# Rest tokens of v ahead of the fourth row tile, and a ring of four PSUM bank pairs for the u and spatial products

## What is computed

```python
kv = einsum('bhsd,bhde->...', k, v); o = q @ kv             # linear attention, no softmax
x  = o / sqrt(mean(o*o, -1) + 1e-6) * g_norm                # 8 heads x 64 -> 512 features
h  = max(x @ w_in, 0);  u, v = h[..., :512], h[..., 512:]
v_n = (v - mean(v)) / sqrt(var(v) + 1e-6)
v_s = einsum('ts,bsd->btd', w_spatial, v_n) + b_spatial     # mixes the 576 tokens
y  = (u * v_s) @ w_out
h2 = max(y @ w_in2, 0);  c = depthwise_conv3(h2)
out = (h2 * sigmoid(c)) @ w_out2
```

## Time and profile before

| | |
|---|---|
| time, median of 3 runs | 794.38 us (793.95 to 794.77) |
| the profiled execution's own time, and its span | 794.56 us, 792.5 us |
| PE busy | 781.0 us, 99% of the span |
| PE weight load busy | 702.0 us, 89% |
| DVE busy | 584.9 us, 74% |
| ACT busy | 421.9 us, 53% |
| POOL busy | 29.5 us, 4% |
| granted TensorE clock | 1.00 |
| chain that ended last | PE 89%, DVE 6%, DMA 1%, ACT 1%, issue 1% |

### The profile page before, as it was taken

One profiled execution on the slowest core, in us unless ns is written; L12 is line 12 of the kernel. 1 busy time (PEld: TensorE's weight loads), 2 busy tenths in 40 slices (PEclk: granted clock), 3 DMA queues, 4 the chain that ended last, 5 costly groups with the idle time before them and its releaser, 6 DMA issues.

```text
span 792.5 us, 15400 instructions
## 1 busy us (share of the span) xinstructions
PE 781.0 (99%) x5654; PEld 702.0 (89%) x5654; DVE 584.9 (74%) x1262; ACT 421.9 (53%) x753; POOL 29.5 (4%) x40
## 2 busy tenths in 40 slices
PE   8999999999999999999999999999999999999997
PEld 7679889798988979899899898898989999898986
DVE  3666776776577475666889989497995979679791
ACT  3664462544335254352556767366674756557562
POOL 4342000000000000000000000000000000000000
PEclk9999999999999999999999999999999999999999
DMA  9872455856334272222091213222022212102101
GB/s 316 308 256 61 150 199 193 301 181 224 105 103 181 74 268 60 104 51 80 36 355 67 105 54 105 67 75 84 1 105 67 104 53 86 71 13 105 53 0 66
DMA packets 35001, 96.86 MB, mean 122 GB/s; under 512 B 2738, under 2 KB 9106, under 8 KB 30228
## 3 DMA queue, kind: packets, MB, share of 16 engines
q1 hardware_dynamic: 33476, 90.09, 33.2%
q10 hardware_dynamic: 1488, 6.30, 2.1%
HBM read 66.11 MB, written 30.28 MB: 122 GB/s over the span
## 4 chain that ended last, share of the span: by engine, by line
PE 89%; DVE 6%; DMA 1%; ACT 1%; issue 1%; SPq 0%; DVEq 0%; ACTq 0%
PE ps L619 25%; PE ps L443 24%; PE ps L611 21%; PE ps L474 11%; PE ps L396 3%; PE ps L412 2%; PE ps L544 1%; DMA kv_raw<-kv_rest_dram 1%; PE ps L422 1%; DVE t_then_s L1148 1%; DVE bn_stats L1067 1%; DVE work L1087 1%; DVE v_hg_split L1093 1%; DVE vrr L1080 0%; PE ps L532 0%
## 5 line engine op out<-in xcount | busy, mean ns | idle before, releaser
L619 PE MATMUL ps<-w_in_split,v_hg_split 128*128 128x512 f32 x832 | 194.9, 390 | 0.0
L619 PEld LDWEIGHTS ps<-w_in_split,v_hg_split 128*128 128x128 f32 x832 | 155.7, 188 | 32.2
L443 PE MATMUL ps<-w_sp_split,v_hg_split 128*128 128x288 f32 x896 | 120.5, 295 | 1.0 <-DVE v_hg_split L1095 0.6
L443 PEld LDWEIGHTS ps<-w_sp_split,v_hg_split 128*128 128x128 f32 x896 | 119.3, 188 | 1.5 <-issue 0.8
L443 PE MATMUL ps<-x_operand_split,w_in_split 128*128 128x288 f32 x768 | 104.3, 296 | 1.6 <-ACT work L701 1.6
L443 PEld LDWEIGHTS ps<-x_operand_split,w_in_split 128*128 128x128 f32 x768 | 102.1, 188 | 3.7 <-ACT work L701 2.0
L474 PE MATMUL ps<-w_in_split,x_operand_split 128*128 128x512 f32 x384 | 93.6, 397 | 0.0
L474 PEld LDWEIGHTS ps<-w_in_split,x_operand_split 128*128 128x128 f32 x384 | 70.4, 188 | 20.9 <-issue 6.1
L1244 DVE TENSOR_TENSOR h_and_sums<-h_and_sums,ps 128x288 f32<-128x288 f32 x160 | 68.5, 450 | 7.5 <-PE ps L611 7.2
L1100 DVE TENSOR_TENSOR work<-ps,work 128x576 f32<-128x576 f32 x32 | 24.1, 757 | 59.4 <-PE ps L443 59.1
L1244 DVE TENSOR_TENSOR h_and_sums<-work,ps 128x288 f32<-128x288 f32 x64 | 28.2, 450 | 46.8 <-PE ps L611 46.3
(11 more groups left out here) (123 smaller groups left out, 1035.9 us busy)
## 6 DMA issues: line engine op xcount, KB each, us to landing
kv_raw<-kv_main_dram SPq DMA_DIRECT2D x8, 2048.0 KB, 10.2
q_raw<-q_T_dram SPq DMA_DIRECT2D x8, 1152.0 KB, 7.2
operand_scratch<-t_then_s SPq DMA_DIRECT2D x8, 1152.0 KB, 5.3
operand_raw<-operand_scratch SPq DMA_DIRECT2D x8, 1152.0 KB, 5.5
sq_then_r<-r_scratch SPq DMA_DIRECT2D x14, 576.0 KB, 6.2
operand_scratch<-work SPq DMA_DIRECT2D x24, 288.0 KB, 2.6
operand_more_raw<-operand_scratch SPq DMA_DIRECT2D x8, 864.0 KB, 7.2
w_out_split_scratch<-v_hg_split ACTq DMA_DIRECT2D x2, 2048.0 KB, 9.0
```

Source lines behind the costliest of these rows:

```text
L443: last = pe.matmul(pair[bank][:, c, :], st, mo[:, c * HALF:(c + 1) * HALF], start=(n == 0), stop=(n == len(steps) - 1))
L619: last = pe.matmul(PS[:, ROW_BANK[i], :], x, wout2[:, w, F_ORDER[e], :], start=(e == 0 and n == 0), stop=(e == FT - 1 and n == len(PASSES) ...
```

## The change

The positions of the v tiles become a list, `V_TILES`, and everything on ACT and DVE that counted by tile counts by position. The rest tokens stand at position 3 and tile 3 at position 4. The rest product writes bank 0 in place of bank 2. A fourth pair (banks 6 and 7) is added; u product and spatial product m = 0 use it, and the others move on by one. The waits follow from the banks: u product 0 waits for nothing more, u product 1 for four `v_relu`s, 2 for all five, and 3 for what 2 waited for before; spatial product 0 waits for one `u_relu` in place of two, 1 for all four in place of three, 2 and 3 for nothing more. The last matmul of v tile 2 gets two waits that stood ahead of the rest product in another form.

```diff
-U_PAIR = [0, 1, 2, 0]
-GATE_PAIR = [1, 2, 0, 1]
+U_PAIR = [3, 0, 1, 2]
+GATE_PAIR = [3, 2, 0, 1]
-V_BANK = [0, 1, 2, 3, 2]
+V_TILES = [0, 1, 2, FULL, 3]
+V_BANK = [0, 1, 2, 3, 0]
-        pair = [PS[:, 2 * i:2 * i + 2, 0:HALF] for i in range(3)]
+        pair = [PS[:, 2 * i:2 * i + 2, 0:HALF] for i in range(4)]
             def v_product(b, i, ahead):
-                if i == FULL:
-                    pe.wait_ge(s_xr, b + 1)
-                    pe.wait_ge(s_vr, b * NT + 3)
+                steps = [(m, a, w) for m in range(MT) for a, w in PASSES]
+                for n, (m, a, w) in enumerate(steps):
+                    if n == len(steps) - 1:
+                        if i == 2:
+                            pe.wait_ge(s_xr, b + 1)
+                            pe.wait_ge(s_vr, b * NT + 1)
+                        if ahead:
+                            if i == 0:
+                                o_ready(b + 1, 1)
+                            if i == 2:
+                                o_ready(b + 1, 3)
+                            if i == 3:
+                                square_ready(b + 1)
+            def v_rest_product(b):
+                steps = [(m, w) for m in range(MT) for w in (HI, LO)]
+                for n, (m, w) in enumerate(steps):
+                    last = pe.matmul(PS[:, V_BANK[FULL], 0:F1], x_rest[:, m, :], WA[:, w, m, F1:2 * F1],
+                                     start=(n == 0), stop=(n == len(steps) - 1))
+                last.then_inc(s_v, 1)
             def u_product(b, m, ahead):
-                if m == 0:
-                    pe.wait_ge(s_vr, b * NT + 2)
-                elif m == 1:
-                    pe.wait_ge(s_vr, (b + 1) * NT)
-                elif m == 2:
-                    if ahead:
-                        pe.wait_ge(s_ms, b + 2)
-                else:
-                    pe.wait_ge(s_ur, b * MT + 1)
+                if m == 1:
+                    pe.wait_ge(s_vr, b * NT + 4)
+                elif m == 2:
+                    pe.wait_ge(s_vr, (b + 1) * NT)
+                elif m == 3 and ahead:
+                    pe.wait_ge(s_ms, b + 2)
             def spatial_product(b, m):
                 if m == 0:
                     pe.wait_ge(s_vlo, (b + 1) * NT)
-                if m < 3:
-                    pe.wait_ge(s_ur, b * MT + 2 + m)
-                else:
-                    pe.wait_ge(s_g, b * MT + 1)
+                    pe.wait_ge(s_ur, b * MT + 1)
+                if m == 1:
+                    pe.wait_ge(s_ur, b * MT + 4)
# PE, body
-                for i in range(NT):
+                for i in V_TILES:
+                    if i == FULL:
+                        v_rest_product(b)
+                        continue
                     v_product(b, i, ahead)
# ACT and DVE: v_relu, v_root, v_hi, v_stats, v_normalise, v_lo (b, i) -> (b, p), for example
-                    act.activation(v_sb[i % 2], src, ACT.Relu).then_inc(s_vr, 1)
+                    act.activation(v, src, ACT.Relu).then_inc(s_vr, 1)      # i, v = V_TILES[p], v_sb[p % 2]
```

More of the change, by code:

```diff
@@ L445, in wide, with v_product @@
                 return last
-            def v_product(b, i, ahead=True):
+            def v_product(b, i, ahead):
                 if i == 0:
@@ L466, in v_product @@
[L466 to L469, removed]
-                        if i == 2:
[L471 to L474, removed]
+                steps = [(m, a, w) for m in range(MT) for a, w in PASSES]
@@ new lines, in v_product @@
+                for n, (m, a, w) in enumerate(steps):
+                    if n == len(steps) - 1:
+                        if i == 2:
+                            pe.wait_ge(s_xr, b + 1)
[7 more added lines that the diff above has]
+                                square_ready(b + 1)
+                    last = pe.matmul(PS[:, V_BANK[i], 0:F1], XG[:, a, m, i * P:(i + 1) * P], WA[:, w, m, F1:2 * F1],
+                                     start=(n == 0), stop=(n == len(steps) - 1))
@@ L700, in v_relu, with v_root, v_hi @@
                     act.wait_ge(s_vsum, b + 1)
[L701 to L705, removed]
+                    act.activation(v[0:REST, :], v[0:REST, :], ACT.Relu).then_inc(s_vr, 1)
+            def v_root(b, p):
+                n = P if V_TILES[p] < FULL else REST
+                act.wait_ge(s_ve, b * NT + p + 1)
                 act.activation(vsd[0:n, :], ve[0:n, :], ACT.Sqrt).then_inc(s_vsd, 1)
-            def v_hi(b, i):
-                act.wait_ge(s_vn, b * NT + i + 1)
+            def v_hi(b, p):
+                i, v = V_TILES[p], v_sb[p % 2]
+                act.wait_ge(s_vn, b * NT + p + 1)
                 if i < FULL:
-                    act.activation(vn[:, HI, i, :], v_sb[i % 2], ACT.Copy).then_inc(s_vhi, 1)
+                    act.activation(vn[:, HI, i, :], v, ACT.Copy).then_inc(s_vhi, 1)
                 else:
-                    act.activation(vnB[0:REST, :], v_sb[0][0:REST, :], ACT.Copy)
-                    act.activation(vnA[0:REST, :], v_sb[0][0:REST, :], ACT.Copy).then_inc(s_vhi, 1)
+                    act.activation(vnB[0:REST, :], v[0:REST, :], ACT.Copy)
+                    act.activation(vnA[0:REST, :], v[0:REST, :], ACT.Copy).then_inc(s_vhi, 1)
             def u_relu(b, m):
@@ L738, in body @@
                         sp_hi(i - 2)
-                    if ahead and i == FULL:
+                    if ahead and i == NT - 1:
                         root(b + 1)
@@ L1059, in wo2_low, with v_stats, v_normalise @@
                 dve.tensor_tensor(wo2_lo[:, f, :], wo2_raw[:, f, :], wo2_hi[:, f, :].bitcast(F32), ALU.subtract).then_inc(s_wo2, 1)
[L1061 to L1063 removed]
+            def v_stats(b, p):
+                n = P if V_TILES[p] < FULL else REST
+                if n == REST:
                     dve.wait_ge(s_vtmp, b + 1)
[L1065 to L1068, removed]
+                    dve.tensor_tensor(v_sb[p % 2][0:n, :], PS[0:n, V_BANK[FULL], 0:F1], v_rest, ALU.add).then_inc(s_vsum, 1)
+                dve.wait_ge(s_vr, b * NT + p + 1)
+                dve.bn_stats(stats[0:n, :], v_sb[p % 2][0:n, :]).then_inc(s_vst, 1)
+                dve.wait_ge(s_vst, (b * NT + p) * 2 + 1)
                 dve.tensor_copy(carrier[0:n, :], stats[0:n, 1:2])
                 dve.bn_aggr(mv[0:n, :], stats[0:n, :]).then_inc(s_vst, 1)
[L1071 removed]
+                dve.wait_ge(s_vst, (b * NT + p) * 2 + 2)
                 dve.tensor_scalar(ve[0:n, :], mv[0:n, 1:2], EPS, None, ALU.add).then_inc(s_ve, 1)
[L1074 to L1077, removed]
+            def v_normalise(b, p):
+                n = P if V_TILES[p] < FULL else REST
+                c = (b * NT + p) * 4
+                dve.wait_ge(s_vsd, b * NT + p + 1)
                 dve.reciprocal(vr0[0:n, :], vsd[0:n, :]).then_inc(s_vrs, 1)
@@ L1086, in v_normalise, with v_lo @@
                 dve.wait_ge(s_vrs, c + 4)
-                dve.tensor_scalar(v_sb[i % 2][0:n, :], v_sb[i % 2][0:n, :], mv[0:n, 0:1], vrs[0:n, :],
+                dve.tensor_scalar(v_sb[p % 2][0:n, :], v_sb[p % 2][0:n, :], mv[0:n, 0:1], vrs[0:n, :],
                                   ALU.subtract, ALU.mult).then_inc(s_vn, 1)
-            def v_lo(b, i):
-                dve.wait_ge(s_vhi, b * NT + i + 1)
+            def v_lo(b, p):
+                i, v = V_TILES[p], v_sb[p % 2]
+                dve.wait_ge(s_vhi, b * NT + p + 1)
                 if i < FULL:
-                    dve.tensor_tensor(vn[:, LO, i, :], v_sb[i % 2], vn[:, HI, i, :].bitcast(F32), ALU.subtract).then_inc(s_vlo, 1)
+                    dve.tensor_tensor(vn[:, LO, i, :], v, vn[:, HI, i, :].bitcast(F32), ALU.subtract).then_inc(s_vlo, 1)
                 else:
-                    dve.tensor_tensor(vnA[REST:P, :], v_sb[0][0:REST, :], vnA[0:REST, :].bitcast(F32), ALU.subtract).then_inc(s_vlo, 1)
+                    dve.tensor_tensor(vnA[REST:P, :], v[0:REST, :], vnA[0:REST, :].bitcast(F32), ALU.subtract).then_inc(s_vlo, 1)
             def gate(b, m):
```

17 lines of the change are left out of this document (6 added, 11 removed).

## The result

| | before | changed |
|---|---|---|
| median of 21 runs | 794.56 us (793.95 to 796.78) | 797.09 us (795.34 to 798.03) |
| the profiled execution's own time, its span | 794.56 us, 792.5 us | 795.51 us, 793.5 us |

A forecast was written before the change was run, and what follows sets the result against it. PE was taken to bound the kernel. Batch 0 -0.2, batches 1 to 6 0 and batch 7 +1.2 gave +1.0 us on 794.56, 795.6, or 795.4 us as median; range 794.2 to 796.9 us.

The forecast's parts named there:

- Batches 1 to 6, 0 us: Loop batches: three waits get later conditions, each still met in time with 2.6 us or more in hand; 0 us lost.
- Batch 7, u product 1: Last batch: the rest tile's relu is done 1.9 us before PE arrives, so the 1.02 us wait goes.
- Batch 7, DVE chain, -0.3 us: Last batch: second copy at the end goes (0.54), `v_lo(3)` waits 0.2; last subtraction begins at 391.0 instead of 391.31.
- Batch 7, spatial 1, +1.2 us, pause 2.8: Last batch: spatial 1 waits for `u_relu` 3 behind a `weight_hi`; PE resumes 1.2 us later, pause grows from 0.5 to 2.8.
- Batch 0, -0.2 us: First batch: u product 1's wait goes, but spatial 0 hangs on the DVE chain, taken as 0.2 us earlier.
- its bounds: Batch 0's limits around the -0.2 us: -0.5 and +0.6 us.
- DVE was first at the ports: Batch 0: DVE assumed ready before POOL's subtraction, chain as now; if POOL came first, some 0.45 us more.
- the 0.25 taken: Batch 0: `inverse_root` waits for ACT's root behind two rest copies, not one; between 0 and 0.54 us, 0.25 taken.
- the 0.43 forecast: Batch 0: second copy goes, but DVE has the `b_spatial` row; of 1.18 us only about 0.43 go.
- The sum: Whole kernel: batch 0, batches 1 to 6 and batch 7 together, +1.0 us.
- PE's clock falls in the pause of batch 7: Rival, 399.4 to 402.2 in batch 7: one slow stretch costs 1.7 us more, +2.7 in all, 797.1 us; chance 0.09.
- pauses of 0.9 to 1.7 us did nothing: Argument against the clock rival: PE's longest earlier pause behind its start-up was 1.7 us, with granted clock 1.00.

The follow-up runs named there:

- ring-alone run: Kernel before with the ring of four pairs and its waits alone, v tiles in the old order; median 798.15 us, five runs, all low.
- early relus: Changed kernel with u_relu 2 and 3 of batch 7 right behind u_relu 1 on ACT, ahead of the third weight_hi; 793.21 us, ratio 0.998.
- failed edit of `inverse_root`: Changed kernel with u_relu 2 and 3 moved early in batch 7, plus batch 0's inverse_root on DVE behind the last normalisation; 794.28 us.
- filled pause: Changed kernel with 20 matmuls whose sums nobody reads ahead of spatial product 1's wait in batch 7; 796.16 us, one of 12 runs low.
- 1.8 us in batch 7: Changed kernel with the fourth u_relu ahead of weight_hi A11 on ACT, shortening batch 7's pause; median 796.31 us, 8 of 12 low.
- 2.9 us in batch 0: Changed kernel with u_relu 2 and 3 moved early in batch 7, and ACT's last v copy of batch 0 made three times; 795.93 us, ten of 12 low.
- the order alone: Changed kernel's v tile order with the old ring of three pairs and its waits; 795.04 us, ratio 1.0009, four of eleven low.
- early relus on the kernel before: Kernel before with only u_relu 2 and 3 of batch 7 moved right behind u_relu 1 on ACT; 794.17 us, ratio 0.9986.

## Why the prediction was right, and where it was not

**Batches 1 to 6, 0 us:** right, six pieces of 27.8 us.

**Batch 7, u product 1:** right. The wait is gone, and u product and spatial 0 follow at once.

**Batch 7, DVE chain, -0.3 us:** right within 0.1. The last subtraction starts at 390.91 in place of 391.31, and 0.2 of the 0.4 is that the batch began earlier; `u_relu` 3, 401.30 in place of 401.80, comes 0.3 us sooner when that is taken out.

**Batch 7, spatial 1, +1.2 us, pause 2.8:** right: 401.99 - 401.01 = 0.98, plus the 0.2 by which the batch began sooner, 1.2; the pause 2.74 by the profile. The ring-alone run shows that it is the ring, the early relus that it is the place of `u_relu` 3 on ACT's queue.

**Batch 0, -0.2 us:** the size was off by 0.3. From the first `kv_product` to that of batch 1 it is 88.18 - 15.61 = 72.57 us before and 87.97 - 15.30 = 72.67 after, +0.1, inside its bounds. DVE was first at the ports, as assumed. The traces split the 0.1, counted from the first `kv_product`: the inverse root's reciprocal came 0.3 us later, about the 0.25 taken; from the subtraction behind the inverse root to the row of `b_spatial` it was 2.13 us in place of 1.97, which the sum didn't have; and from that row to the last subtraction 0.78 in place of 1.18, 0.40 of the 0.43 forecast.

**The sum:** +1.0 forecast, +1.3 measured in the first stage of the profiled execution, where the clock did not fall. That the span came out at +1.0 exactly is luck: its start was 0.3 us earlier. The range ended at 796.9 us; the ratio puts the change at 796.4 on the scale of the forecast, inside it, while the median of 797.09 us as it stands is above it.

**The step that failed** is the chance of the rival "PE's clock falls in the pause of batch 7", 0.09. It was put in the right place and near the right price (1.7 by my estimate, 1.3 to 1.5 measured), and by the mean clock it happened in 11 of 21 executions. That its end, 797.1 us, is the very median is luck: the executions with a fall have a median of 797.6, and only the mixture of both groups lies at 797.1. I argued "pauses of 0.9 to 1.7 us did nothing" from one profile of before. One execution can't show that: timed beside the kernels above, the kernel before itself has 12 low runs in 88, at 795.6 to 797.5 us. It was also a mistake to treat the fall as yes or no for the kernel. It is drawn anew in each execution, so a pause adds a share of 1.5 us to the mean and, once that share passes a half, the whole of it to the median. With that chance at one half, my estimate from the same sum would have been 796 to 797 us and "slower" the likeliest sign. The two runs of the changed kernel differ in the share as well, 11 of 21 and 10 of 12.

The Trainium skill ("TensorE: Matmul & The Clock Gate", HAM oscillation) has waits between bursts as the reason for such falls; the windows at 0.50 behind the pauses agree with it. The other page that I drew on ("SBUF — State Buffer", Who interferes with whom) gave two values for batch 0 by which engine issues first. DVE issued first and POOL was held up (1.88 us in place of 1.64), and the failed edit of `inverse_root` showed the stretched steps where it put them.

**What stays open.** Why 1.65 us of idle time in batch 0 lowered the clock in at most one of 23 runs (filled pause and early relus), when 1.8 us in batch 7 did in 8 of 12. The two differ by little in length, and 2.9 us in batch 0 did do it. Nor do I know where the kernel before falls. The three kernels with early relus (on both, and with the later inverse root) had no low run in 33, which points to batch 7. But the wait for `u_relu` 2 or 3 can't be all of it: the order alone had none in its profile, and four of its eleven runs were low, while early relus on the kernel before left a wait of 0.88 us there and none of eleven was. The share of low runs of the kernel before also differs by the set of runs, from one of 27 to four of 15, so small counts say little across sets. No profile of before with a fall was taken.

## What to carry to other kernels

Before a bank ring is lengthened, ask for every bank which reader now frees it and what stands ahead of that reader on its queue, in the unrolled first and last turns above all: the loop here gained nothing, and the last turn lost, where ACT has other work between two relus. Removing a wait that stands ahead of another one only makes the second longer, and a longer pause of PE has a price of its own, since the clock may fall in it or behind it (10 of 12 executions here with the pause of 2.7 us, one of 12 with the same pause filled). So join what remains of a wait with the cure for its cause: here moving two relus ahead of three weight splits turned a loss of 1.3 us in the first stage into a gain of 1.7 (396.65 to 394.98 us).

## What the runs showed of the hardware

Counted by the mean clock, a kernel with a pause of PE of 1.8 us in batch 7 had low runs in 8 of 12 executions, with one of 2.7 us in 21 of 33, with one of 3.0 or 3.7 us in all eleven; where the fall lay is known for the profiled ones alone, and the kernel before, with no pause over 0.9 us in that batch, had 12 in 88. The low stretch lasted about 3.4 us at 0.50 in all five profiles that had one, began from inside the pause to 1.4 us behind it, and cost 1.3 to 1.5 us where it lay in batch 7. Matmuls that nobody needs, put in the pause, kept the clock up in 11 of 12 runs. A mean clock of 0.998 in the result of a run is the sign of it, though the profile taken may show none.
